# Routing searches with whole-array counts and broadcasts, 16-bit comparison tables with the token groups innermost, and high products first at the start of layer three

## The chip, the core and the metric

The kernel runs on one core of a Trainium2 chip. The metric is the device time of one execution in microseconds (us). TensorE (PE in the rows; PEld is its weight load) multiplies, VectorE is DVE, ScalarE is ACT, GpSimd is POOL, and SyncE (SP) issues most DMAs. The kernel before took 959.31 us, the median of three runs (948.09 to 986.38).

## What is computed

The reference runs three stages, cut here to what matters:

```python
# 1. attention, 4 x 8 heads, 576 positions, 64 wide -> x of 2304 tokens x 512 (pooled + local part)
# 2. expert routing and two layers (N, D, E, F = 2304, 512, 8, 1024; cap = 288)
logits = x @ w_gate
order = np.argsort(-logits.flatten())
for idx in order:                          # greedy: best score first
    tok, e = idx // E, idx % E
    if assigned[tok] >= 0 or counts[e] >= cap: continue
    assigned[tok] = e; counts[e] += 1
for e in range(E):
    h = np.maximum(x[assigned == e] @ w1[e], 0.0)
    out[assigned == e] = h @ w2[e]
# 3. two more layers (d_ff = 2048)
h = out @ w_in
g = np.maximum(h, 0.0) + alpha * np.minimum(h, 0.0)
return g @ w_out
```

## The kernel before

**Stages.** Attention fills the first 210 us. Then the router finds the expert that fills up first and the list of its 288 tokens, those rows of x are gathered, and a pass runs all four layers on them. There are eight passes, one for each expert in the order in which they fill. The routing for the first pass stands alone ahead of it; the routing for pass k + 1 is cut into pieces that stand between the matrix products of pass k (`pe_route` on TensorE, `dve_route` and `dve_prepare` on VectorE). The places are a fixed list of half steps (`PLACES`, `ROUTE`).

**Routing.** A token's best open score is a 32-bit key. The router searches for the score at which an expert fills in six levels of digits (5, 5, 5, 5, 6, 6 bits). At a level VectorE writes the table `at_least` (it lies in the buffer `onehot`): for each of 18 token groups and each of 32 or 64 candidate digits, is the token's digit at least this one (L1169). TensorE sums it over the 128 partitions, a **count** of 18 matmuls of bf16 with the weights `choice[:, t, :]`, 128 x 8 (L954), so the result has 8 rows, one per expert. VectorE compares the counts with the free places (`enough`, 8 rows, L1171), and a **broadcast**, one matmul with `ones[0:E, :]`, 8 x 128 (L957), tells all partitions how many experts have enough. VectorE adds this up (L1165) and forms the next place (L1166, L1167). After the levels come one count of everything (L959), two prefix sums (L962), and the **id list**: VectorE writes `onehot`, slot number against token, in two halves (L1234), and 18 matmuls with `onehot[:, t, :]`, 128 x 128, as weights give the token numbers (L965). In the routing that stands alone VectorE also makes the low halves of two resident weight units after each `at_least` (L1351).

**Passes.** Each float32 product is made from high and low halves: `three` issues high x high, low x high, high x low (L936 to L938); `two_by_high` issues the first two (L941, L942), `one_by_low` the third (L945). Layer one and two have 8 hidden blocks (288 columns), layer three and four 16 (256 columns, in passes 3 and 7 384 columns; passes are numbered from 0). Layer two's result y is copied by ScalarE (`y_hi`, L1442), and VectorE subtracts for the low half (`y_lo`, L1259), one chunk of four at a time. Block j of layer three (`pe_third`) goes into one of two PSUM banks. VectorE turns it into `act` in two operations (`dve_third`: `neg`, L1273, then `act`, L1275), ScalarE rounds it (L1446), VectorE makes the low half (`dve_third_low`, L1281), and `pe_fourth` adds the block into the outputs two steps later. Block j >= 2 of layer three waits for `act` of block j - 2. At the end of a pass blocks of 128 tokens are copied out of PSUM and scattered by GpSimd's indirect DMAs, one block after another (`dve_output`, `scatter`).

**Order around the change.** Engines work strictly in the order in which the functions issue. In step s of layers three and four TensorE's order is block s of layer three, a routing piece, block s - 2 of layer four, a routing piece. At s = 0 the piece is the count of the last level, at s = 1 its broadcast. VectorE's order at s = 0 is `neg`, `act` of block 0, then `enough`. Ahead of the four `y_lo` it has the last level's `at_least`.

## Time and profile before

| | before |
|---|---|
| median of three runs, us | 959.31 (948.09 to 986.38) |
| profiled execution, us | 948.44 |
| its span, us (first to last instruction) | 946.7 |
| mean granted TensorE clock, share of full | 0.941 |
| PE busy, us (share of the span) | 883.0 (93%) |
| PEld busy | 785.6 (83%) |
| DVE busy | 646.4 (68%) |
| ACT busy | 329.5 (35%) |
| POOL busy | 144.0 (15%) |
| PE in the chain of work that ended last | 86% |

In the page the span is cut into 40 slices of 23.7 us; a digit is the busy share of a slice in tenths, and PEclk is the clock that TensorE was granted, in tenths of full speed. A matmul's end in these profiles is modelled; what a stretch of matmuls costs is read from the starts of the ones around it.

### The profile page before, as it was taken

The page shows a single profiled execution, that of the slowest core. Times are in us where ns is not written, and L with a number is a line of the kernel's source. Part 1 is how long each engine was busy: PE and PEld are TensorE (multiplying, and loading weights), DVE is VectorE, ACT ScalarE, POOL GpSimd, SP SyncE. Part 2 cuts the span into 40 slices and gives each one's busy share as a digit, 9 for nine tenths or more (in the row PEclk, how much of TensorE's full clock was granted, in tenths as well). Part 3 has the DMA queues.
Part 4 walks back from the last instruction along what each step waited for, and adds up shares of the span by engine and source line. Part 5 has one row for each costly group of instructions (what it writes and reads, how often), then busy time and mean ns, then how long its engine had stood idle before and what let it go on. Part 6 is the DMA issues. An engine that isn't in the chain of part 4 may idle for free.

```text
span 946.7 us, 19340 instructions
## 1 busy us (share of the span) xinstructions
PE 883.0 (93%) x7228; PEld 785.6 (83%) x7228; DVE 646.4 (68%) x1818; ACT 329.5 (35%) x1041; POOL 144.0 (15%) x182
## 2 busy tenths in 40 slices
PE   7999999982299999999999999999999999999996
PEld 7688878771298889999899989898898998999995
DVE  4475858448778976877787766667777877775432
ACT  2666777733154143123214211331241142143111
POOL 4653736310100010010011001100100110020001
PEclk9589999775599999999999999999999999999998
DMA  7666471014453340212213020302122130231000
GB/s 161 150 145 173 103 173 49 19 52 134 136 166 114 100 141 2 89 55 90 90 35 113 1 90 26 111 13 90 52 90 85 37 112 1 90 109 37 1 1 34
DMA packets 122629, 77.29 MB, mean 82 GB/s; under 512 B 64232, under 2 KB 105192, under 8 KB 122536
## 3 DMA queue, kind: packets, MB, share of 16 engines
q1 hardware_dynamic: 119368, 65.83, 25.2%
q0 software_dynamic: 3168, 10.23, 3.4%
q8 instruction: 58, 0.95, 0.4%
q14 instruction: 35, 0.29, 0.1%
HBM read 66.59 MB, written 9.44 MB: 80 GB/s over the span
## 4 chain that ended last, share of the span: by engine, by line
PE 86%; DVE 7%; ACT 3%; issue 2%; DMA 1%; SPq 1%; POOL 0%; DVEq 0%; ACTq 0%; POOLq 0%
PE banks L936 22%; PE banks L937 20%; PE banks L938 20%; PE banks L954 3%; PE banks L258 3%; PE banks L307 2%; PE banks L359 2%; PE banks L270 2%; PE banks L330 2%; ACT prob L527 2%; PE banks L945 1%; PE banks L301 1%; PE banks L980 1%; PE banks L345 1%; PE banks L371 1%
## 5 line engine op out<-in xcount | busy, mean ns | idle before, releaser
L1446 ACT CAST hid<-act 128x256 fp32r<-128x256 f32 (+1 forms) x128 | 55.5, 434 | 326.5 <-DVE act L1275 326.5
L936 PE MATMUL banks<-xy,win 128*128 128x256 f32 (+1 forms) x480 | 143.9, 300 | 0.0
L938 PE MATMUL banks<-xy,win 128*128 128x256 f32 (+1 forms) x480 | 142.1, 296 | 0.0
L937 PE MATMUL banks<-xy,win 128*128 128x256 f32 (+1 forms) x480 | 142.0, 296 | 0.0
L1273 DVE TENSOR_SCALAR neg<-banks,alph 128x256 f32<-128x256 f32 (+1 forms) x128 | 66.1, 517 | 93.7 <-PE banks L938 81.5
L936 PE MATMUL banks<-wout,hid 128*128 128x512 f32 x288 | 116.2, 403 | 0.5 <-DVE hid L1281 0.5
L937 PE MATMUL banks<-wout,hid 128*128 128x512 f32 x288 | 113.4, 394 | 0.0
L938 PE MATMUL banks<-wout,hid 128*128 128x512 f32 x288 | 112.8, 392 | 0.0
L1481 POOL DMA_INDIRECT rows<-x_rows,id_new x24 | 23.2, 966 | 514.6 <-DVE id_new L1240 509.7
L936 PEld LDWEIGHTS banks<-xy,win 128*128 128x128 f32 x480 | 91.2, 190 | 4.9
L937 PEld LDWEIGHTS banks<-xy,win 128*128 128x128 f32 x480 | 91.2, 190 | 3.9
L527 ACT ACTIVATE prob<-banks,nbias 96x102 f32<-96x102 f32 (+1 forms) x256 | 85.9, 351 | 15.4 <-DVE nbias L444 8.1
L938 PEld LDWEIGHTS banks<-xy,win 128*128 128x128 f32 x480 | 91.1, 190 | 0.0
L936 PE MATMUL banks<-hid,w2s 128*128 128x288 f32 x256 | 79.8, 312 | 0.0
L937 PE MATMUL banks<-hid,w2s 128*128 128x288 f32 x256 | 75.3, 294 | 0.0
L938 PE MATMUL banks<-hid,w2s 128*128 128x288 f32 x256 | 75.2, 294 | 0.0
L588 POOL TENSOR_TENSOR prob<-prob,inverse 96x408 f32<-96x408 f32 (+1 forms) x80 | 61.2, 784 | 85.9 <-DVE inverse L461 85.9
L936 PE MATMUL banks<-xy,w1s 128*128 128x288 f32 x224 | 69.6, 311 | 0.1
L1351 DVE TENSOR_TENSOR w2s<-raw,w2s 128x512 fp32r<-128x512 f32 x64 | 44.0, 687 | 33.8 <-ACT w2s L1415 33.8
L937 PE MATMUL banks<-xy,w1s 128*128 128x288 f32 x224 | 66.6, 297 | 0.0
L938 PE MATMUL banks<-xy,w1s 128*128 128x288 f32 x224 | 66.5, 297 | 0.0
L938 PEld LDWEIGHTS banks<-wout,hid 128*128 128x128 f32 x288 | 54.1, 188 | 12.1
(202 smaller groups left out, 1892.9 us busy)
## 6 DMA issues: line engine op xcount, KB each, us to landing
raw<-in_moe_w SPq DMA_DIRECT2D x128, 256.0 KB, 3.3
qn<-in_q SPq DMA_DIRECT2D x48, 96.0 KB, 2.5
kn<-in_k SPq DMA_DIRECT2D x48, 96.0 KB, 2.5
vn<-in_v SPq DMA_DIRECT2D x4, 1152.0 KB
x_rows<-xs SPq DMA_DIRECT2D x24, 192.0 KB, 2.4
raw<-in_moe_w_in SPq DMA_DIRECT2D x16, 256.0 KB, 3.2
raw<-in_moe_w_out SPq DMA_DIRECT2D x16, 256.0 KB, 3.8
vw<-in_v SPq DMA_DIRECT2D x16, 204.0 KB
```

The lines of the kernel that those rows point to most:

```text
L258: nc.tensor.matmul(bank[:, 0:128], ident[:], ident[:], start=True, stop=True)
L270: last = nc.tensor.transpose(bank[:, x * T:(x + 1) * T], (qn, kn)[t][:, c * (R // 2) + x, 2 * hp:2 * hp + 2, :].rearrange("p h d -> p (h d)"),
L527: last = nc.scalar.activation(prob[0:rows, ring, at * width:(at + 1) * width], pS[u % 2][0:rows, g, n * width:(n + 1) * width], ACT.Exp, b ...
L588: nc.gpsimd.tensor_tensor(p, p, inv.unsqueeze(2).to_broadcast([rows, heads, width]), ALU.mult).then_inc(normed, 1)
L936: nc.tensor.matmul(out_ap, a_hi, b_hi, start=start, stop=False)
L937: nc.tensor.matmul(out_ap, a_lo, b_hi, start=False, stop=False)
L938: return nc.tensor.matmul(out_ap, a_hi, b_lo, start=False, stop=stop)
L954: last = nc.tensor.matmul(pR[0:E, 0:radix], choice[:, t, :], at_least[i // 2][:, t, :], start=(t == 0), stop=(t == NT - 1))
L1273: v.tensor_scalar(neg[:, 0:n], pH[j % 2][:, 0:n], 0.0, alph[:, j:j + 1], ALU.min, ALU.mult).then_inc(neg_made, 1)
L1351: v.tensor_tensor(unit_dst(n, resident, 1), raw[:, raw_slot(k, n)[0], :], unit_dst(n, resident, 0).bitcast(F32), ALU.subtract).then_inc(lo ...
L1446: nc.scalar.copy(hid[:, (FC + j) % 3, 0, 0:CHUNK[k]], act[:, j % 2, 0:CHUNK[k]]).then_inc(h_hi, 1)
L1481: nc.gpsimd.indirect_dma_start(out=rows[0:n, j, :], out_offset=None, in_=x_dram, in_offset=bass.IndirectOffsetOnAxis(ap=id_new[0:n, j:j + ...
```

## The change

- **Counts.** `choice` becomes the front of a wider, zero-filled buffer `choice_all`, and the weights of each count matmul are its 128 columns from t * E on: the first 8 are the group's, the other 120 give rows that nobody reads. The tile is 128 x 128 where it was 128 x 8.
- **Broadcasts.** `enough` has 128 rows, those behind the eighth zero, and the weights are all of `ones`: 128 x 128 where it was 8 x 128.
- **16-bit data, groups innermost.** `place`, the slot numbers (`slot16`), `any_v` and one table of numbers (`number`, 128 x 128 x 18) are bf16. `at_least` and `onehot` lie with the 18 groups innermost. So both inputs and the output of L1169 and L1234 are 16-bit with step 1, and TensorE reads `at_least[:, :, t]` (moving) and `onehot[:, :, t]` (weights) with a step of 18 elements, 36 bytes.
- **Layer three.** Blocks 0 and 1: the high products of both, then the low ones of block 0, the last count, the low ones of block 1.
- **`neg`** is written into `act` itself, so `dve_third` also waits for the low half of block j - 2.
- **Last pass.** The last two blocks of layer four are run together, token block by token block (`pe_fourth_last`).
- **Start.** The memsets of the routing's buffers move to the front of VectorE's program, with two new ones; VectorE waits for `logits` by semaphore. GpSimd fills `number` (2304 numbers a partition) where it filled 64 and 128.

```diff
-    f["digit_at"] = sb("digit_at", [T, J], F32)
-    f["slot_at"] = sb("slot_at", [T, SLOTS], F32)
+    f["number"] = sb("number", [T, SLOTS, NT], BF16)
...
-    choice = sb("choice", [T, NT, E], BF16)
+    choice_all = sb("choice", [T, NT * E + T - E], BF16)
...
-    place = sb("place", [T, 2, NT], F32)
-    enough = sb("enough", [E, J], BF16)
-    any_v = sb("any_v", [T, J], F32)
+    place = sb("place", [T, 2, NT], BF16)
+    slot16 = sb("slot16", [T, NT], BF16)
+    enough = sb("enough", [T, J], BF16)
+    any_v = sb("any_v", [T, J], BF16)
...
-    onehot = sb("onehot", [T, NT, SLOTS], BF16)
+    onehot = sb("onehot", [T, SLOTS, NT], BF16)
...
-                    last = nc.tensor.matmul(pR[0:E, 0:radix], choice[:, t, :], at_least[i // 2][:, t, :],
+                    last = nc.tensor.matmul(pR[:, 0:radix], choice_all[:, t * E:t * E + T], at_least[i // 2][:, :, t],
                                             start=(t == 0), stop=(t == NT - 1))
             else:
-                last = nc.tensor.matmul(pR[0:T, 0:radix], f["ones"][0:E, :], enough[:, 0:radix], start=True, stop=True)
+                last = nc.tensor.matmul(pR[0:T, 0:radix], f["ones"][:], enough[:, 0:radix], start=True, stop=True)
...
-                last = nc.tensor.matmul(pR[0:SLOTS, 0:2 * JT], onehot[:, t, :], ids[:, t].rearrange("p a b -> p (a b)"),
+                last = nc.tensor.matmul(pR[0:SLOTS, 0:2 * JT], onehot[:, :, t], ids[:, t].rearrange("p a b -> p (a b)"),
...
+    def pe_third_by_high(e, k, j):
+
+        e.wait_ge(h_lo, k * NC + FC + j + 1)
...
+            two_by_high(pH[j % 2][:, 0:CHUNK[k]], win[:, 0, j, c, :], win[:, 1, j, c, :], xy[:, 0, c, 0:CHUNK[k]], c == 0)
+
+    def pe_third_by_low(e, k, j):
...
+            last = one_by_low(pH[j % 2][:, 0:CHUNK[k]], win[:, 0, j, c, :], xy[:, 1, c, 0:CHUNK[k]], c == DC - 1)
+        last.then_inc(h_in_psum, 1)
...
+    def pe_fourth_last(e, k):
+
+        for i in range(BLOCKS[k]):
+            tokens = slice(i * SLOTS, (i + 1) * SLOTS)
+            for j in (FC2 - 2, FC2 - 1):
+                if i == 0:
+                    e.wait_ge(h_lo, k * NC + FC + j + 1 + 2)
+                r = (FC + j) % 3
+                last = three(pY[i], hid[:, r, 0, tokens], hid[:, r, 1, tokens], wout[:, 0, j, :], wout[:, 1, j, :],
+                             False, j == FC2 - 1)
+            last.then_inc(o_in_psum, 1)
...
-            if s < FC2:
+            if s == 0:
+                pe_third_by_high(e, k, 0)
+                pe_third_by_high(e, k, 1)
+                pe_third_by_low(e, k, 0)
+            elif s == 1:
+                pe_third_by_low(e, k, 1)
+            elif s < FC2:
                 pe_third(e, k, s)
...
-                each = [T, NT, radix]
-                ask(v.tensor_tensor(at_least[l], bc(here, 2, each), bc(f["digit_at"][:, 0:radix], 1, each), ALU.is_ge))
+                ask(v.tensor_tensor(at_least[l], bc(here, 1, [T, radix, NT]), f["number"][:, 0:radix, :], ALU.is_ge))
...
-            ins = v.tensor_tensor(onehot[:, h], bc(slot[:, h], 2, half), bc(f["slot_at"][:], 1, half), ALU.is_equal)
+            ins = v.tensor_tensor(onehot[:, h], bc(slot16[:], 1, [T, SLOTS // 2, NT]), f["number"][:, h], ALU.is_equal)
...
-        v.tensor_scalar(neg[:, 0:n], pH[j % 2][:, 0:n], 0.0, alph[:, j:j + 1], ALU.min, ALU.mult).then_inc(neg_made, 1)
+        e.wait_ge(h_lo, k * NC + FC + j + 1)
+        v.tensor_scalar(act[:, j % 2, 0:n], pH[j % 2][:, 0:n], 0.0, alph[:, j:j + 1], ALU.min, ALU.mult).then_inc(neg_made, 1)
```

TensorE's program at the start of layer three in pass 0, before: matmuls of layer three read `win`, the row with `choice` is the last count, the row with `enough` its broadcast; the high products of block 0 stand ahead of the first row.

```order
L942 MATMUL banks<-xy,win 128x256
L945 MATMUL banks<-xy,win 128x256 x4
L954 MATMUL banks<-onehot,choice 8x64 x18
L936 MATMUL banks<-xy,win 128x256
L937 MATMUL banks<-xy,win 128x256
L938 MATMUL banks<-xy,win 128x256
...
L957 MATMUL banks<-enough,ones 128x64
L936 MATMUL banks<-xy,win 128x256
```

The same place after the change, where the helper lines are one lower:

```order
L941 MATMUL banks<-xy,win 128x256
L944 MATMUL banks<-xy,win 128x256 x4
L953 MATMUL banks<-onehot,choice 128x64 x18
L944 MATMUL banks<-xy,win 128x256 x4
L956 MATMUL banks<-enough,ones 128x64
L935 MATMUL banks<-xy,win 128x256
```

Ahead of the count stand now 16 high products in place of 8, and between count and broadcast 4 matmuls in place of 12.

VectorE's program at a level of the routing that stands alone, a piece of before and the same piece of after; `win` and `wout` are the low halves of two resident weight units:

```order
L1169 TENSOR_TENSOR onehot<-place,digit_at 128x1152
L1351 TENSOR_TENSOR win<-raw,win 128x512
L1351 TENSOR_TENSOR wout<-raw,wout 128x512
L1171 TENSOR_SCALAR enough<-banks,cap 8x64
```

```order
L1195 TENSOR_TENSOR onehot<-place,number 128x1152
L1377 TENSOR_TENSOR win<-raw,win 128x512
L1377 TENSOR_TENSOR wout<-raw,wout 128x512
L1197 TENSOR_SCALAR enough<-banks,cap 8x64
```

Nothing has moved here: the two weight operations stand between the table and `enough` as before, and only the table's operands differ.

## Rows read from the trace of the kernel before

**Rows 1.** The page: the clock granted to TensorE in the 40 slices.

```profile
PEclk9589999775599999999999999999999999999998
```

**Rows 2.** Waits of TensorE, 205 to 262 us, then 262 to 946 us: total us, times, longest us.

```profile
PE banks L954 <- DVE onehot L1169: 14.9, 6, 5.8
...
PE banks L954 <- DVE onehot L1169: 0.6, 1, 0.6
```

**Rows 3.** Groups by line on VectorE: output<-inputs, shapes, count, busy us, mean ns.

```profile
L1169 DVE TENSOR_TENSOR onehot<-place,digit_at 128x576 bf16<-128x576 f32 x32 | 24.2, 756 | 0.9
L1169 DVE TENSOR_TENSOR onehot<-place,digit_at 128x1152 bf16<-128x1152 f32 x16 | 21.7, 1358 | 0.6
```

**Rows 4.** Timeline of the routing that stands alone, a 64-column count: start us, length us.

```profile
229.79 1.12 PE L954 MATMUL banks<-onehot,choice 128*8 128x64 bf16 x18 [2.17 <-DVE onehot L1169]
```

**Rows 5.** Timeline of TensorE in pass 1, around a 64-column count.

```profile
369.32 0.29 PE L938 MATMUL banks<-hid,w2s 128*128 128x288 f32 x1
369.60 0.69 PE L954 MATMUL banks<-onehot,choice 128*8 128x64 bf16 x18
...
370.45 0.29 PE L937 MATMUL banks<-hid,w2s 128*128 128x288 f32 x1
370.58 0.29 PE L938 MATMUL banks<-hid,w2s 128*128 128x288 f32 x1
```

**Rows 6.** Timeline of TensorE in pass 1, around a 32-column count.

```profile
357.70 0.29 PE L938 MATMUL banks<-hid,w2s 128*128 128x288 f32 x1
357.92 0.60 PE L954 MATMUL banks<-onehot,choice 128*8 128x32 bf16 x18
...
358.69 0.30 PE L937 MATMUL banks<-xy,w1s 128*128 128x288 f32 x1
```

**Rows 7.** Timeline of TensorE in pass 1, around bf16 pieces with 128 x 128 weights.

```profile
381.23 0.39 PE L938 MATMUL banks<-wout,hid 128*128 128x512 f32 x1
381.46 0.30 PE L959 MATMUL banks<-choice,ones 128*128 128x288 bf16 x1
...
381.71 0.28 PE L937 MATMUL banks<-xy,win 128*128 128x256 f32 x1
...
405.69 0.28 PE L938 MATMUL banks<-xy,win 128*128 128x256 f32 x1
405.81 0.61 PE L965 MATMUL banks<-ids,onehot 128*128 128x6 bf16 x18
...
406.59 0.39 PE L937 MATMUL banks<-wout,hid 128*128 128x512 f32 x1
```

**Rows 8.** Timeline of pass 1 where layer three begins, VectorE and TensorE.

```profile
372.98 1.36 DVE L1169 TENSOR_TENSOR onehot<-place,digit_at 128x1152 bf16<-128x1152 f32 x1
373.81 0.28 PE L941 MATMUL banks<-xy,win 128*128 128x256 f32 x1
374.26 1.54 DVE L1259 TENSOR_TENSOR xy<-banks,xy 128x288 fp32r<-128x288 f32 x4
374.80 1.44 PE L945 MATMUL banks<-xy,win 128*128 128x256 f32 x4
376.38 0.48 DVE L1273 TENSOR_SCALAR neg<-banks,alph 128x256 f32<-128x256 f32 x1 [0.32 <-PE banks L945]
377.24 0.26 DVE L1171 TENSOR_SCALAR enough<-banks,cap 8x64 bf16<-8x64 f32 x1
378.21 0.28 PE L938 MATMUL banks<-xy,win 128*128 128x256 f32 x1
378.42 0.20 PE L957 MATMUL banks<-enough,ones 8*128 8x64 bf16 x1
378.77 0.28 PE L937 MATMUL banks<-xy,win 128*128 128x256 f32 x1
```

**Rows 9.** Timeline of GpSimd at the end of the span: the first and the last scatter.

```profile
937.44 0.97 POOL L1491 DMA_INDIRECT out<-rows,id_now  x1 [89.87 <-DVE rows L1302]
...
940.00 0.97 POOL L1491 DMA_INDIRECT out<-rows,id_now  x1 [0.30 <-issue]
```

More of the change, by code:

```diff
@@ L727, in early_buffers, with experts @@
     alph = sb("alph", [128, FC2], F32)
-    return (open_l, best, pick, pick_n, choice, free, flip, key, digits_i, digits, place, enough, any_v, reach,
+    return (open_l, best, pick, pick_n, choice_all, free, flip, key, digits_i, digits, place, enough, any_v, reach,
             over_t, tie, choice2, taken, need, room, cap8, cap_d, penalty, full, fullest, sel, junk, expert_f,
-            expert_i, need1, mine, tied, upto, rowsum, rank, take, member, gone, mem, past, slot, in_tile, ids,
+            expert_i, need1, mine, tied, upto, rowsum, rank, take, member, gone, mem, past, slot, slot16, in_tile, ids,
             onehot, id_parts, id_f, id_new, id_now, id_left, raw, alph)
-def experts(nc, logits, w1, w2, w_in, w_out, alpha, x_dram, out, ident, f, early, consts_made, n_consts, TILE, SLOTS, psum, sem, sb, over):
+def experts(nc, logits, w1, w2, w_in, w_out, alpha, x_dram, out, ident, f, early, consts_made, n_consts, TILE, SLOTS, psum, sem, sb, over, logits_known):
     E, DM, F = w1.shape
@@ L750, in experts @@
     assert CAP * E == N and LEFT[E] == 0 and max(LEFT) + CAP <= WIDE <= 3 * SLOTS and min(BLOCKS) >= 2 and DM == 512 and FC % 2 == 0
-    J = f["digit_at"].shape[1]
+    J = 1 << max(DIGIT_BITS)
     LEVELS = len(DIGIT_BITS)
@@ L777, in experts @@
     hid = sb("hid", [128, 3, 2, WIDE], F32R)
-    neg = sb("neg", [128, WIDE], F32)
     act = sb("act", [128, 2, WIDE], F32)
     rows = sb("rows", [SLOTS, JT, DM], F32)
-    (open_l, best, pick, pick_n, choice, free, flip, key, digits_i, digits, place, enough, any_v, reach,
+    (open_l, best, pick, pick_n, choice_all, free, flip, key, digits_i, digits, place, enough, any_v, reach,
      over_t, tie, choice2, taken, need, room, cap8, cap_d, penalty, full, fullest, sel, junk, expert_f,
-     expert_i, need1, mine, tied, upto, rowsum, rank, take, member, gone, mem, past, slot, in_tile, ids,
+     expert_i, need1, mine, tied, upto, rowsum, rank, take, member, gone, mem, past, slot, slot16, in_tile, ids,
      onehot, id_parts, id_f, id_new, id_now, id_left, raw, alph) = early
     prod = pick
-    flat_onehot = onehot[:].rearrange("p t m -> p (t m)")
-    at_least = [flat_onehot[:, 0:NT * j].rearrange("p (t j) -> p t j", t=NT) for j in RADIX]
+    choice = choice_all[:, 0:NT * E].rearrange("p (t e) -> p t e", e=E)
+    flat_onehot = onehot[:].rearrange("p m t -> p (m t)")
+    at_least = [flat_onehot[:, 0:NT * j].rearrange("p (j t) -> p j t", t=NT) for j in RADIX]
     pH = [psum[0], psum[1]]
@@ L1016, in pe_second @@
             last.then_inc(h_used, 1)
[L1018 to L1024 removed]
+    def pe_third_by_high(e, k, j):
+        e.wait_ge(h_lo, k * NC + FC + j + 1)
+        if k == 0:
+            wait_low(e, None, 2 * j)
+        if j == 0 and LEFT[k] > 0:
+            e.wait_ge(left_hi, lefts_to(k))
+        for c in range(DC):
+            if j == 0:
+                e.wait_ge(y_hi, k * DC + c + 1)
+            two_by_high(pH[j % 2][:, 0:CHUNK[k]], win[:, 0, j, c, :], win[:, 1, j, c, :], xy[:, 0, c, 0:CHUNK[k]], c == 0)
+    def pe_third_by_low(e, k, j):
+        if j == 0 and LEFT[k] > 0:
+            e.wait_ge(left_lo, lefts_to(k))
+        for c in range(DC):
+            if j == 0:
+                e.wait_ge(y_lo, k * DC + c + 1)
+            last = one_by_low(pH[j % 2][:, 0:CHUNK[k]], win[:, 0, j, c, :], xy[:, 1, c, 0:CHUNK[k]], c == DC - 1)
+        last.then_inc(h_in_psum, 1)
+    def pe_third(e, k, j):
+        e.wait_ge(act_made, k * FC2 + j - 1)
+        if k == 0:
             wait_low(e, None, 2 * j)
         out_ap, y = pH[j % 2][:, 0:CHUNK[k]], xy[:, :, :, 0:CHUNK[k]]
[L1027 to L1039 removed]
+        for c in range(DC):
+            last = three(out_ap, win[:, 0, j, c, :], win[:, 1, j, c, :], y[:, 0, c, :], y[:, 1, c, :], c == 0, c == DC - 1)
         last.then_inc(h_in_psum, 1)
@@ L1076, in pe_pass @@
                 pe_turn(e, k + 1, 1)
-            if s >= DELAY:
+            if s >= DELAY and (more or s < SECOND - 2):
                 pe_fourth(e, k, s - DELAY)
+            if not more and s == SECOND - 2:
+                pe_fourth_last(e, k)
             if more and at + 1 in pe_piece:
@@ L1352, in dve_weights, with vector_begin @@
                         ALU.subtract).then_inc(lo_by_dve, 1)
-    def vector(e):
-        e.sem_inc(h_lo, 2)
+    def vector_begin(e):
+        v.memset(enough[:], 0.0).then_inc(begun, 1)
+        v.memset(choice_all[:], 0.0).then_inc(begun, 1)
         v.memset(free[:], 1.0).then_inc(begun, 1)
```

56 lines of the change are left out of this document (21 added, 35 removed).

## The prediction

> **What bounds the kernel now.** I read the slices of the page first, then TensorE's waits, then the timeline of one pass. The page gives TensorE 93% of the span and 86% of the chain that ended last. Its clock stands at half (1.2 of 2.4 GHz) in the two slices of the routing that stands alone, and at full from there on [rows 1]. In that stretch TensorE waits for VectorE: six waits of 14.9 us in all for the tables of the six levels. From 262 us to the end the same wait occurs once, with 0.6 us [rows 2]. So there are two regimes. In the routing that stands alone, some 48 us, VectorE's chain of operations sets the time. In the eight passes, 676 us, TensorE has no gap, and every piece that stands between the products costs what it takes on TensorE. What it takes is read from the starts of the products around it, since a matmul's modelled length overlaps with the next.
>
> **The counts and broadcasts in the passes.** Products of 288 columns start 0.13 us apart, those of 256 columns 0.12 and those of 512 columns 0.23 [rows 5, 7, 8]. Around a 64-column count the product before starts at 369.32 and the second one behind it at 370.45: 1.13 us, less two steps of 0.13, leaves 0.87 us for the piece [rows 5]. A 32-column count costs 358.69 - 357.70 - 0.26 = 0.73 us [rows 6]. A broadcast, one matmul of 64 columns, costs 378.77 - 378.21 - 0.24 = 0.32 us [rows 8]. The pieces whose tile is already 128 x 128 are much cheaper: one bf16 matmul of 288 columns costs 381.71 - 381.23 - 0.23 - 0.12 = 0.13 us, and the 18 of the id list 406.59 - 405.69 - 0.12 - 0.23 = 0.55 us [rows 7]. Both are bf16 between float32 products and start without a gap, so the extra is not due to the type; the broadcast has the same 128 columns of weights and only 8 rows, so what it has in common with the counts is a tile smaller than the array. I take the price after from these pieces. Broadcast: 0.13, a gain of 0.19. 32-column count: 18 matmuls as in the id list, 0.56, a gain of 0.17. 64-column count: 0.09 more, the difference of the two counts' lengths of 0.69 and 0.60 [rows 5, 6], so 0.64, a gain of 0.23. Routing is mixed into seven passes, with four small counts, two large ones and six broadcasts each: 28 x 0.17 + 14 x 0.23 + 42 x 0.19 = 4.8 + 3.2 + 8.0 = 16.0 us. The bound on the good side is a count with nothing but its columns. The one on the bad side is the new step of 36 bytes, which no row shows. The nearest row is the same count at half the clock, 1.12 us for 18 [rows 4], against 0.69 [rows 5]: if the strided read ran at half rate, a large count would cost 0.43 more, and a small one, whose 32 columns then take no longer than 64 do now, 0.09 at most. I take no penalty, since the rows nearest in form (18 matmuls, 128 x 128) are of the packed kind and nothing in them is bound by reading.
>
> The Trainium skill speaks against this (Advanced Engine Details and Errata, section SBUF Cachelines): at least two accesses must hit a line of 16 bytes for full rate, and a step of 36 bytes gives one. By that rule the large counts would keep little of their gain; no row here has such a step on TensorE.
>
> **The tables on VectorE.** `at_least` takes 0.756 us for 576 elements and 1.358 for 1152 [rows 3]. The difference is 0.602 for 576, so the fixed part is 0.154. With 16-bit data throughout it lies between the fixed part and today's price; no row of `tensor_tensor` has only 16-bit operands. I take the middle, half the price per element: 0.455 and 0.756, a gain of 0.30 and 0.60. In the routing that stands alone these are on the path. At level 0 the gain is lost, and with it that of the memsets that move to the front: `enough` stands there behind weight units that wait for their DMA. Levels 1 to 3 give 3 x 0.30, since the small count is shorter than the two weight operations behind the table. Levels 4 and 5 give 2 x 0.60 if the large count stays at its 1.12 us [rows 4]: it starts earlier with the table and ends about when the two weight operations do, as now. The two halves of `onehot`, of the larger shape, give 1.2. Sum 3.3 us. If the clock rises at the same instant as now although the first pass starts 3.3 us sooner, half of it goes again: bounds 1.7 and 3.3, none at all if 16-bit data are no faster. In pass 0 the one wait for a table [rows 2] goes: 0.6 us. In the other passes a faster table is worth nothing by itself, since TensorE does not wait for it.
>
> The Trainium skill (VectorE: DVE Perf Modes, section The perf-mode tier table) has `tensor_tensor` on bf16 in SBUF at two elements a cycle. By that page the two tables would take about 0.46 and 0.76 us, an estimate, and the gain would be the same.
>
> **Layer three.** Before, TensorE starts the high products of block 0 at 373.81, its low ones at 374.80, and they last 1.44 us to 376.24 in place of four steps, because `y_lo` runs only from 374.26 to 375.80, behind the last table of 1.36 us. `neg` starts 0.14 us behind the last low product, `enough` 0.86 us behind `neg`, takes 0.26, and the broadcast starts at 378.42 [rows 8]. After: high products of both blocks to 374.80 + 0.96 = 375.76, the last of four low ones starts at 376.12 and ends at 376.40, 0.16 later than now; `neg` 376.54, `enough` 377.40 to 377.66, the broadcast about 377.72. TensorE itself would be ready at 375.76 + 0.48 + 0.64 + 0.48 = 377.36. So the wait on `y_lo` goes and a new wait of 0.4 us for `enough` comes. The broadcast is 0.70 earlier, of which the count's 0.23 is booked already: 0.45 us in each of six passes, 2.7 us. In pass 3, with 384 columns, the chain behind block 0 is longer by two operations of 128 more columns, 0.27 us, and little was waited for: I take -0.2. Pass 7 has no routing: block 2 waits for `act` of block 0. That is ready 1.0 us behind the end of block 0's last product, as `enough` is ready to start [rows 8], 0.1 more until `act` has ended, 0.27 for the columns and 0.16 for the product's own end; four products of 0.17 cover 0.7 of the 1.5 us: -0.8 us. Sum 1.7 us; bounds -1 and 4. What a faster table does here is hidden: with `y_lo` 0.6 us sooner the old order would have lost its stall too, so the new order by itself is then worth less than nothing, some 0.3 us a pass.
>
> **The rest.** In the last pass the first token block is complete after 6 of the last 18 products where it was after 12: 6 x 0.23 = 1.4 us earlier. The three scatters are issued one after another, 1.28 us apart, from 937.44 to 940.00 [rows 9], so the last issue moves as far as the first, unless its own copy, which does not move, holds it: I take 1.2 us, an estimate (bounds 0 and 1.4). `neg` in place and its wait cost nothing: the operation it waits for stands just ahead of it on VectorE, which mostly waits for TensorE there. The memsets and the longer fill of `number`, some 2 us of GpSimd, lie in the first microseconds, where VectorE and GpSimd wait for inputs.
>
> **Sum.** 16.0 + 3.3 + 0.6 + 1.7 + 1.2 = 22.8 us, against the profiled execution's 948.44: 925.6, I say 926 us. The median of the runs shown lies 1.1% above that execution and its lowest run at 948.09; the sum is for an execution like the profiled one, and the range's upper part has to hold a median that lies higher.
>
> **The rivals.**
> - *The strided reads run at half rate.* For it: the step lets each element be read alone, where two stand together now. Against it: pieces of 18 matmuls take 0.55 us for 6 columns and 0.73 for 32, so columns are hardly what bounds them [rows 6, 7]. It costs 14 x 0.43 = 6.0 us in the large counts, and if the weights of the id list load at half rate too, about 0.45 us in each of eight, 3.6 us: 935 us. Chance 0.28.
> - *16-bit data are no faster on VectorE*, because of the repeated row of `place`: 3.3 and 0.6 us are lost, 929.5 us. Chance 0.10.
> - *The new wait in layer three is longer than 0.4 us*, because `act` and `enough` come later than worked out. At 1 us more in each pass: 934 us. Chance 0.07.
> - *Slower than before.* The place is TensorE's read with the 36-byte step, in all 42 counts and 7 id lists of the passes. The gain is gone when each costs 22.8 / 49 = 0.47 us more, that is 26 ns a matmul, twice the present step; slower by 2% needs 0.85 us each. A half rate does not do this to the small counts. Chance 0.05.
>
> **How the numbers follow.** My forecast has 0.50. Its own range is 920 to 931, by the bounds of the terms. Half rate ends at 935 and the longer wait at 934, and a median above an undisturbed execution adds up to 1%, so the range is 918 to 940. A measurement of this kernel can tell about 2% from no change. Faster by over 2% means below 929.5: most of the forecast (0.42) and a part of the VectorE and half-rate cases (0.08), 0.50. Slower by over 2%: 0.04. Within: 0.46.
>
> **What would show it.** A broadcast piece should cost 0.13 us between the starts around it, a small count 0.56, a large one 0.64, and a pass of 256 columns should be 2.7 us shorter. The tables should take 0.46 and 0.76 us. TensorE should wait 0.4 us for `enough` ahead of the last broadcast, and 0.8 us in the last pass ahead of block 2. I am wrong if the count pieces are as dear as now (the step), if the tables keep 0.76 and 1.36 us, or if the pieces with a full tile owe their low price to something else.

## The result

The changed kernel takes 980.44 us (median of 4 runs, 975.75 to 983.91); the kernel before, on the same chip, 960.55 (4 runs, 948.09 to 986.38). The ratio is 1.025 with a 95% interval of 1.014 to 1.036: slower, though not surely by over 2%, where 926 us and a gain had been forecast. Ratios and intervals here leave out executions over 1.5% above the fastest of their kernel; medians leave out none. The profiled execution took 983.91 us, the longest of the four, with a span of 982.2 us, 35.5 us more than the span before.

The page of the changed kernel: engines, and the granted clock in 40 slices.

```profile
span 982.2 us, 19390 instructions
PE 921.4 (94%) x7228; PEld 835.7 (85%) x7228; DVE 621.7 (63%) x1820; ACT 331.2 (34%) x1041; POOL 146.7 (15%) x181
PEclk9595988975589999999999999999999999999999
```

Groups of the changed kernel by line, engine and shape (count, then busy us, mean ns of one, idle ahead): the count, its weights, the id list, its weights; and the tables on VectorE.

```profile
L953 PE MATMUL banks<-onehot,choice 128*128 128x32 bf16 x576 | 39.9, 239 | 9.0 <-DVE onehot L1195 9.0
L953 PE MATMUL banks<-onehot,choice 128*128 128x64 bf16 x288 | 36.2, 295 | 3.4 <-DVE onehot L1195 3.4
L964 PE MATMUL banks<-ids,onehot 128*128 128x6 bf16 x144 | 10.2, 204 | 3.7 <-DVE onehot L1259 3.7
...
L964 PEld LDWEIGHTS banks<-ids,onehot 128*128 128x128 bf16 x144 | 9.6, 160 | 4.2 <-DVE onehot L1259 3.8 <-issue 0.2
...
L1195 DVE TENSOR_TENSOR onehot<-place,number 128x576 bf16<-128x576 bf16 x32 | 14.6, 456 | 0.9
L1195 DVE TENSOR_TENSOR onehot<-place,number 128x1152 bf16<-128x1152 bf16 x16 | 12.1, 758 | 0.5
```

The tables came out as forecast, 456 and 758 ns where [rows 3] has 756 and 1358. The counts did not, as TensorE's timeline of pass 1 shows: a small count, a large count, an id list (start us, length us). They answer to [rows 5] to [rows 8].

```profile
381.36 0.29 PE L937 MATMUL banks<-xy,w1s 128*128 128x288 f32 x1
381.49 1.25 PE L953 MATMUL banks<-onehot,choice 128*128 128x32 bf16 x18
...
382.76 0.29 PE L936 MATMUL banks<-hid,w2s 128*128 128x288 f32 x1
...
387.39 0.29 PE L937 MATMUL banks<-hid,w2s 128*128 128x288 f32 x1
387.52 2.26 PE L953 MATMUL banks<-onehot,choice 128*128 128x64 bf16 x18
...
389.76 0.29 PE L936 MATMUL banks<-hid,w2s 128*128 128x288 f32 x1
...
425.19 0.28 PE L937 MATMUL banks<-xy,win 128*128 128x256 f32 x1
425.31 1.28 PE L964 MATMUL banks<-ids,onehot 128*128 128x6 bf16 x18
...
426.78 0.39 PE L936 MATMUL banks<-wout,hid 128*128 128x512 f32 x1
```

By starts, as before: the large count costs 389.76 - 387.39 - 0.26 = 2.11 us (0.87 before, 0.64 forecast), the small one 382.76 - 381.36 - 0.26 = 1.14 (0.73, 0.56), the id list 426.78 - 425.19 - 0.12 - 0.23 = 1.24 (0.55, unchanged by the forecast). The broadcasts cost 0.12 to 0.13 on average, as forecast. Against a packed full tile, a pass then pays 4 x 0.59 + 2 x 1.47 + 0.69 = 6.0 us more.

**Where the time lies.** The routing that stands alone begins with `open_l` at 210.93 us before and at 224.74 after, although nothing ahead of it was changed but memsets, the fill of `number` and one wait. VectorE's timeline, before, then after:

```profile
210.93 0.31 DVE L1122 TENSOR_TENSOR open_l<-logits,penalty 128x144 f32<-128x144 f32 x1
```

```profile
224.74 0.31 DVE L1149 TENSOR_TENSOR open_l<-logits,penalty 128x144 f32<-128x144 f32 x1
```

So 13.8 of the 35.5 us lie ahead of all that the change is about, and from this start to the end of the span it is 735.8 us before and 757.5 after, 21.7 more. I use this "rest" for all kernels below; it repeats within 0.4 us in the three kernels that were profiled twice. Between kernels it is less sharp: e6's pieces cost what the changed kernel's do, and its passes 1 to 6 agree to 0.05 us, yet its routing and pass 0 together take 2.9 us more (138.3 against 135.4), for which no cause was found. A price is therefore read from passes 1 to 6. Stages, us:

| kernel | routing begins | first product behind it | pass 1 | pass 3 | last pass, to its last matmul | rest |
|---|---|---|---|---|---|---|
| before | 210.9 | +47.0 | 79.99 | 101.44 | 92.64 | 735.8 |
| e4 (before again) | 210.4 | +47.8 | 79.99 | 101.44 | 92.67 | 735.8 |
| changed | 224.7 | +48.8 | 83.02 | 104.88 | 93.56 | 757.5 |
| e10 (changed again) | 216.3 | +48.2 | 83.01 | 104.88 | 93.62 | 757.1 |
| e1, packed (2 bytes) | 212.5 | +48.7 | 77.68 | 99.72 | 93.58 | 722.3 |
| e2, pairs (4 bytes) | 213.7 | +44.6 | 77.34 | 99.38 | 93.58 | 714.1 |
| e9 (6 bytes) | 238.1 | +46.3 | 77.67 | 99.70 | 93.58 | 719.0 |
| e5 (12 bytes) | 230.4 | +46.5 | 80.69 | 102.58 | 93.62 | 738.6 |
| e6 (18 bytes) | 218.7 | +49.3 | 83.01 | 104.89 | 93.60 | 760.5 |
| e7, 36 bytes, narrow tile | 221.9 | +48.6 | 84.40 | 106.35 | 93.61 | 767.6 |
| e3, broadcasts alone | 225.9 | +47.9 | 79.19 | 100.60 | 92.65 | 731.3 |
| e8, pairs, old layer three | 226.3 | +45.2 | 77.28 | 98.93 | 92.67 | 713.6 |
| e12 (e8 again) | 230.9 | +45.5 | 77.26 | 98.93 | 92.67 | 713.4 |
| e11, e8 and old last groups | 205.6 | +45.7 | 77.29 | 98.93 | 92.66 | 714.8 |

### The profile page after: what moved, and what is told of

It is laid out like the page before. It is cut to its first block, busy times and chain, and to the rows that moved or that the text cites. A ratio compares the mean times of both kernels' runs of the same rounds, so it can differ in the third digit from the quotient of the medians.

```text
span 982.2 us, 19390 instructions
## 1 busy us (share of the span) xinstructions
PE 921.4 (94%) x7228; PEld 835.7 (85%) x7228; DVE 621.7 (63%) x1820; ACT 331.2 (34%) x1041; POOL 146.7 (15%) x181
## 4 chain that ended last, share of the span: by engine, by line
PE 84%; SPq 6%; DVE 3%; DMA 2%; ACT 2%; issue 1%; POOL 0%; ACTq 0%; POOLq 0%; DVEq 0%
PE banks L935 20%; PE banks L936 19%; PE banks L937 19%; PE banks L953 7%; SPq L201 4%; PE banks L359 2%; PE banks L307 2%; SPq L211 2%; PE banks L330 2%; PE banks L940 1%; PE banks L270 1%; PE banks L258 1%; PE banks L941 1%; PE banks L944 1%; ACT prob L527 1%
## 5 line engine op out<-in xcount | busy, mean ns | idle before, releaser
L935 PE MATMUL banks<-xy,win 128*128 128x256 f32 (+1 forms) x448 | 133.7, 299 | 0.6 <-DVE act L1301 0.6
L1299 DVE TENSOR_SCALAR act<-banks,alph 128x256 f32<-128x256 f32 (+1 forms) x128 | 66.2, 517 | 107.2 <-PE banks L937 85.3
L937 PE MATMUL banks<-xy,win 128*128 128x256 f32 (+1 forms) x448 | 132.8, 296 | 0.0
L936 PE MATMUL banks<-xy,win 128*128 128x256 f32 (+1 forms) x448 | 132.6, 296 | 0.0
L935 PEld LDWEIGHTS banks<-xy,win 128*128 128x128 f32 x448 | 85.2, 190 | 5.1 <-DVE act L1301 0.9
L936 PEld LDWEIGHTS banks<-xy,win 128*128 128x128 f32 x448 | 85.1, 190 | 3.9
L953 PE MATMUL banks<-onehot,choice 128*128 128x32 bf16 (+1 forms) x864 | 76.1, 257 | 12.4 <-DVE onehot L1195 12.4
L937 PEld LDWEIGHTS banks<-xy,win 128*128 128x128 f32 x448 | 85.1, 190 | 0.0
L953 PEld LDWEIGHTS banks<-onehot,choice 128*128 128x128 bf16 x864 | 65.9, 116 | 16.1 <-DVE onehot L1195 8.0
L935 PE MATMUL banks<-xy,w1s 128*128 128x288 f32 x224 | 68.7, 307 | 0.1
L936 PE MATMUL banks<-xy,w1s 128*128 128x288 f32 x224 | 66.2, 296 | 0.0
```

Source lines behind the costliest of these rows:

```text
L935: nc.tensor.matmul(out_ap, a_hi, b_hi, start=start, stop=False)
L936: nc.tensor.matmul(out_ap, a_lo, b_hi, start=False, stop=False)
L937: return nc.tensor.matmul(out_ap, a_hi, b_lo, start=False, stop=stop)
L953: last = nc.tensor.matmul(pR[:, 0:radix], choice_all[:, t * E:t * E + T], at_least[i // 2][:, :, t], start=(t == 0), stop=(t == NT - 1))
L1299: v.tensor_scalar(act[:, j % 2, 0:n], pH[j % 2][:, 0:n], 0.0, alph[:, j:j + 1], ALU.min, ALU.mult).then_inc(neg_made, 1)
```

## Experiments: the step of the reads

Theory: the 36-byte step makes TensorE's reads dear, moving data and weights. Rival: the whole-array tile itself costs it.

**e1_packed**: the changed kernel with the groups outermost again, so that reads are packed; the tables then have a repeated input.

```diff
-    onehot = sb("onehot", [T, SLOTS, NT], BF16)
+    onehot = sb("onehot", [T, NT, SLOTS], BF16)
...
-                    last = nc.tensor.matmul(pR[:, 0:radix], choice_all[:, t * E:t * E + T], at_least[i // 2][:, :, t],
+                    last = nc.tensor.matmul(pR[:, 0:radix], choice_all[:, t * E:t * E + T], at_least[i // 2][:, t, :],
...
-                last = nc.tensor.matmul(pR[0:SLOTS, 0:2 * JT], onehot[:, :, t], ids[:, t].rearrange("p a b -> p (a b)"),
+                last = nc.tensor.matmul(pR[0:SLOTS, 0:2 * JT], onehot[:, t, :], ids[:, t].rearrange("p a b -> p (a b)"),
```

> The changed kernel with one part undone: the tables lie as before, the candidates of a group side by side, so TensorE reads them packed; 16-bit data, whole-array counts and broadcasts and all else stay. Theory S (the step of 36 bytes costs, 1.75 ns a column): a small count falls from 1.15 to about 0.56 us, a large one from 2.11 to about 0.64, the id list from 1.24 to 0.55; a pass of 256 columns takes 77.3 us (83.0 in the changed kernel, 80.0 before), and the kernel is about 19 us faster than before. Theory W (the wide tile itself costs, by its 128 weight columns or 128 result rows): counts stay at 1.15 and 2.11 us and passes near 82.5. The tables on VectorE go back to 0.76 and 1.36 us under both, since one input then repeats one element.

**e2_groups_of_two**: the table in pairs of groups. The reads have a step of 2 elements, 4 bytes, and VectorE has runs of two equal neighbours in all its operands. e9_step6, e5_step12 and e6_step18 are the same with 3, 6 and 9 in place of 2.

```diff
+    onehot = sb("onehot", [T, NT // 2, SLOTS, 2], BF16)
...
+                    last = nc.tensor.matmul(pR[:, 0:radix], choice_all[:, t * E:t * E + T], at_least[i // 2][:, t // 2, :, t % 2],
...
+                last = nc.tensor.matmul(pR[0:SLOTS, 0:2 * JT], onehot[:, t // 2, :, t % 2], ids[:, t].rearrange("p a b -> p (a b)"),
...
+                each = [T, NT // 2, radix, 2]
+                ask(v.tensor_tensor(at_least[l], bc(here.rearrange("p (a g) -> p a g", g=2), 2, each), bc(f["number"][:, 0:radix, :], 1, each), ALU.is_ge))
```

> The changed kernel with another table layout: groups in pairs, [9 pairs][candidates][2], so TensorE reads with a step of 4 bytes where it was 36, and VectorE still has two elements side by side everywhere. If what costs is the distance (a new piece of memory for each column), counts cost 0.56 and 0.64 us, the id list 0.55, tables still 0.46 and 0.76 us, and the kernel is some 22 us faster than before. If every step but one element costs alike, counts stay at 1.15 and 2.11 us and the time at that of the changed kernel. Anything between says how the price grows with the step.

Measured: e1 943.74 us, ratio 0.986 (0.979 to 0.991); e2 928.64, ratio 0.979 (0.965 to 0.993). TensorE's timeline of e2 in pass 1, the small count, the large one and the id list:

```profile
342.21 0.29 PE L937 MATMUL banks<-xy,w1s 128*128 128x288 f32 x1
342.35 0.61 PE L953 MATMUL banks<-onehot,choice 128*128 128x32 bf16 x18
...
343.02 0.29 PE L936 MATMUL banks<-xy,w1s 128*128 128x288 f32 x1
...
363.98 0.29 PE L937 MATMUL banks<-hid,w2s 128*128 128x288 f32 x1
364.11 0.71 PE L953 MATMUL banks<-onehot,choice 128*128 128x64 bf16 x18
...
364.88 0.29 PE L936 MATMUL banks<-hid,w2s 128*128 128x288 f32 x1
...
399.20 0.28 PE L937 MATMUL banks<-xy,win 128*128 128x256 f32 x1
399.32 0.61 PE L964 MATMUL banks<-ids,onehot 128*128 128x6 bf16 x18
...
400.10 0.39 PE L936 MATMUL banks<-wout,hid 128*128 128x512 f32 x1
```

That is 0.55, 0.64 and 0.55 us, the forecast's 0.56, 0.64 and 0.55. With the same full tile as in the changed kernel the counts are cheap again, and by the whole of what was lost: 83.02 - 77.34 = 5.68 us a pass, where the pieces make 6.0 and a wait for `enough`, which e2 has and the changed kernel hardly, takes the 0.3 between them (below). In e1 the tables take 757 and 1358 ns again, as dear as in [rows 3], so both things are shown: on 16-bit data a repeated input keeps VectorE at the old price, and pairs are enough for the new one. Its large count waits 0.34 us for its table. Its passes of 77.68 us came near the 77.3 expected, but its rest is 13.5 us shorter than before and not 19: the old tables cost in the routing too.

One group of e1, the 64-column table on VectorE:

```profile
L1195 DVE TENSOR_TENSOR onehot<-place,number 128x1152 bf16<-128x1152 bf16 x16 | 21.7, 1358 | 0.6
```

VectorE's groups of e2, the tables and the two parts of the slot table:

```profile
L1196 DVE TENSOR_TENSOR onehot<-place,number 128x576 bf16<-128x576 bf16 x32 | 14.6, 456 | 0.9
L1196 DVE TENSOR_TENSOR onehot<-place,number 128x1152 bf16<-128x1152 bf16 x16 | 12.1, 758 | 0.6
L1262 DVE TENSOR_TENSOR onehot<-slot,number 128x1280 bf16<-128x1280 bf16 x8 | 6.6, 819 | 0.0
L1262 DVE TENSOR_TENSOR onehot<-slot,number 128x1024 bf16<-128x1024 bf16 x8 | 5.5, 685 | 0.0
```

**e7_narrow_tile**: the changed kernel with the 36-byte step, but the old count tile of 128 x 8.

```diff
-                    last = nc.tensor.matmul(pR[:, 0:radix], choice_all[:, t * E:t * E + T], at_least[i // 2][:, :, t],
+                    last = nc.tensor.matmul(pR[0:E, 0:radix], choice_all[:, t * E:t * E + E], at_least[i // 2][:, :, t],
```

> The changed kernel with the counts' tile back to 128 x 8 and the step of 36 bytes kept. If the moving read alone costs (1.75 ns a column), a large count stays at 18 x 0.117 = 2.1 us and gets the 0.25 us of the switch of tiles on top, some 2.35 us, a small one 1.4. If the 128 columns of weights take part in the price, the counts get cheaper than 2.11 and 1.15 us.

TensorE's timeline of e7, pass 1, the large count:

```profile
387.10 0.29 PE L937 MATMUL banks<-hid,w2s 128*128 128x288 f32 x1
387.33 2.26 PE L953 MATMUL banks<-onehot,choice 128*8 128x64 bf16 x18
...
389.75 0.30 PE L936 MATMUL banks<-hid,w2s 128*128 128x288 f32 x1
```

Measured: 991.26 us in one execution; the large count costs 2.39 us and the small one 1.36. The narrow tile is dearer by 0.28 and 0.22 us at the 36-byte step too, a little over the 0.23 and 0.17 that the forecast gave the full tile. The rival falls: the tile brought its gain, and the step took it and more.

**How the price goes with the step.**

> The changed kernel with groups in sixes, [3][candidates][6]: TensorE reads with a step of 12 bytes. At 4 bytes a large count costs 0.63 us, at 36 bytes 2.11. Theory L (the price comes from how many columns lie in one stretch of 16 bytes: four at a step of 4, one and a third at 12, one at 36): a large count near the dear end, 1.5 to 2.1 us. Theory D (the price grows evenly with the distance): 0.63 + 8/32 of 1.48 = 1.0 us, a small count 0.70.

> The changed kernel with groups in nines, [2][candidates][9]: a step of 18 bytes. Theory L: every column lies in a stretch of its own, so the price is that of 36 bytes: 2.1 us for a large count, 1.15 for a small one, 1.24 for the id list. Theory D: 0.63 + 14/32 of 1.48 = 1.28 us for a large count. The tables have rows of nine, an odd number; if VectorE still takes two at a time they stay at 0.46 and 0.76 us.

> The changed kernel with its tables in groups of three of the 18: the values that one count matmul reads stand 6 bytes apart (2 bytes in e1_packed, 4 in e2_groups_of_two, 12 in e5_step12, 18 in e6_step18, 36 in the changed kernel). Prices so far at 4, 12 and 18 bytes, from starts around the piece: small count 0.55, 0.90, 1.15 us; large count 0.63, 1.60, 2.13 us; id list 0.55, 0.95, 1.18 us. By the stretch theory (what costs is the number of 16-byte stretches that a row of the read touches, 1.85 ns each, 2.13 us over 18 x 64, and nothing beyond the floor of the packed piece): 3 of 8 values open a new stretch, so the large count takes 18 x 64 x 3/8 x 1.85 ns = 0.80 us, the small one 0.40 us by stretches and so its floor of 0.55 us, the id list its floor of 0.55 us. By the distance theory (an even rise from 4 to 18 bytes): large 0.84, small 0.64, id list 0.64 us. The small count and the id list tell them apart.

Measured: 970.74, 980.88 and 958.81 us for 12, 18 and 6 bytes, one execution each, so with all the chance of the attention stage. By the starts around the pieces, in us (middle of the pieces that started without a wait):

| step, bytes | small count, 576 values | large count, 1152 | id list, 2304 weights | rest |
|---|---|---|---|---|
| 2 | 0.55 | 0.62 | 0.55 | 722.3 |
| 4 | 0.55 | 0.63 | 0.55 | 714.1 |
| 6 | 0.55 | 0.88 | 0.58 | 719.0 |
| 12 | 0.90 | 1.60 | 0.95 | 738.6 |
| 18 | 1.15 | 2.13 | 1.18 | 760.5 |
| 36 | 1.14 | 2.11 | 1.24 | 757.5 |

The rest is not the step's alone: at 2 bytes the tables are slow (e1), and at 6 and 18 bytes their rows of 3 and 9 are odd. VectorE's tables of e9, then of e6:

```profile
L1196 DVE TENSOR_TENSOR onehot<-place,number 128x1152 bf16<-128x1152 bf16 x16 | 15.3, 958 | 0.6
```

```profile
L1196 DVE TENSOR_TENSOR onehot<-place,number 128x1152 bf16<-128x1152 bf16 x16 | 13.2, 825 | 0.6
```

With rows of 2, 6 and 18 they take 758 ns. Less the forecast's fixed 154 ns, 958 is 4/3 and 825 is 10/9 of that: an odd row costs what the next even one does, so e6's tables did not stay at 0.76 us.

The large count at 12 and at 6 bytes, in TensorE's timelines of e5, then of e9:

```profile
386.85 0.29 PE L937 MATMUL banks<-hid,w2s 128*128 128x288 f32 x1
386.98 1.74 PE L953 MATMUL banks<-onehot,choice 128*128 128x64 bf16 x18
...
388.72 0.29 PE L936 MATMUL banks<-hid,w2s 128*128 128x288 f32 x1
```

```profile
391.49 0.29 PE L937 MATMUL banks<-hid,w2s 128*128 128x288 f32 x1
391.63 0.97 PE L953 MATMUL banks<-onehot,choice 128*128 128x64 bf16 x18
...
392.63 0.29 PE L936 MATMUL banks<-hid,w2s 128*128 128x288 f32 x1
```

The price rises from 12 to 18 bytes and no further to 36, so it is not the distance. It goes with the number of 16-byte stretches that a row of the read touches: one for each value at 18 and 36 bytes, 3/4 at 12, 3/8 at 6. With stretches of 8 bytes the price at 12 would be that at 36, with 32 bytes that at 18 would lie below it; neither is so. Between the small and the large count at 18 bytes lie (2.13 - 1.15) / 576 = 1.7 ns for each value, which leaves 0.17 us for the piece. Then 12 bytes give 0.17 + 0.75 x 1.96 = 1.64 (measured 1.60) and 0.91 (0.90), and 6 bytes 0.91 (0.88), while at 4 bytes the stretches come to 0.66, about what a packed piece costs anyhow (0.62). The count's price at 12 and 18 bytes fits the stretches and not an even rise; at 6 bytes e9's expectation of 0.80 for the large count was 0.08 too low since it left the fixed part out, but the small count stayed at 0.55, where an even rise would have given 0.64. The id list, whose strided operand is the weights, behaves alike at a lower price, with the same 0.17 us taken off (1.24 - 0.17) / 2304 = 0.46 ns a stretch. The Trainium skill (Advanced Engine Details and Errata, section SBUF Cachelines) has SBUF in lines of 16 bytes that need at least two hits each; the trace agrees with the line's size. By the two-hit rule a 6-byte step, with two or three hits a line, would be free; the large count at 0.88 against 0.63 is not.

At half the clock it is, as the large counts of e9 and e2 in the routing show (granted clock 0.50 in both):

```profile
257.04 1.14 PE L953 MATMUL banks<-onehot,choice 128*128 128x64 bf16 x18 [1.77 <-DVE onehot L1196]
```

```profile
231.55 1.14 PE L953 MATMUL banks<-onehot,choice 128*128 128x64 bf16 x18 [1.57 <-DVE onehot L1196]
```

Both last 1.14 us there, 0.97 and 0.71 in the passes, while e5's lasts 1.74 in both places. So what a count costs here is the longer of two things: its columns, which go with the clock, and its stretches, which do not.

## Experiments: what else the change did

**e3_broadcast_only**: the kernel before, with nothing but the whole-array broadcasts.

```diff
-    enough = sb("enough", [E, J], BF16)
+    enough = sb("enough", [T, J], BF16)
...
-                last = nc.tensor.matmul(pR[0:T, 0:radix], f["ones"][0:E, :], enough[:, 0:radix], start=True, stop=True)
+                last = nc.tensor.matmul(pR[0:T, 0:radix], f["ones"][:], enough[:, 0:radix], start=True, stop=True)
```

> The kernel before with the broadcasts alone made 128 x 128. If a tile smaller than the array costs the switch, the piece falls from 0.32 to 0.13 us, passes of 256 columns from 80.0 to 78.9 us, and the span's part behind the first product by about 8 us. If the low price of the full pieces came from something else, it stays at 0.32 us and 80.0 us.

**e4_before_again**: the kernel before, unaltered, beside it.

> The kernel before once more, for its attention stage. In the changed kernel's profile the routing began at 224.7 us, in that of before at 210.9. If this is chance (where the clock of TensorE falls to half in attention), this run's start of the routing may lie anywhere from 210 to 225 us, and kernels with the new start of the program may lie anywhere there too. If it is the changed start (memsets and the longer table fill ahead of attention), it stays at about 211 here and at about 224 in the two kernels that keep the new start.

Measured: 958.95 and 947.97 us, one execution each. The broadcast costs 0.13, and pass 1 is 0.80 us shorter, not 6 x 0.19 = 1.1: the large count in it, at 1.05 us by its starts, now waits 0.33 us for its table, as in e1. So the rest is 4.5 us shorter and not 8, and e3 still took longer than e4, since its routing began at 225.9 and not 210.4.

**e10_after_again**: the changed kernel once more, for that start.

> The changed kernel once more, unaltered. The stand-alone routing began at 210.9 us in the profile of the kernel before and at 224.7 us in that of the changed one, with the same attention code ahead of it. If the 13.8 us are chance of the execution (which stretches of attention run at the half clock), the routing begins anywhere between 210 and 231 us here, as it did over the runs so far, while the seven passes and the last one repeat theirs to 0.2 us each but pass 0 (83.0 a pass, 104.9 for pass 3, 93.6 the last). If they belong to the changed program, it begins at 224 to 225 us again.

Measured: 975.16 us. The routing began at 216.27, passes 1 to 6 repeated to 0.03 us and the last one to 0.06. Over all the profiles it began anywhere between 205.6 and 238.1, for one kernel (e8, e12) at 226.3 and 230.9. The granted clock of e11 and of e9, the two ends:

```profile
PEclk9589999995599999999999999999999999999998
```

```profile
PEclk9569556999559999999999999999999999999998
```

Ahead of the routing's own two slices at half clock (5), e11 has one and e9 three, with two more partly so (6). A slice is 23 to 24 us. Kernels with the old start of the program lie as far apart (210.4 and 225.9 for e4 and e3) as those with the new one. So the 13.8 us are chance of the execution, and what decides how much of attention runs at half clock was not settled. That this is also most of the spread of the executions without a trace is likely, not shown.

**e8_pairs_old_third**: e2 with layer three in its old order.

```diff
-            if s == 0:
-                pe_third_by_high(e, k, 0)
-                pe_third_by_high(e, k, 1)
-                pe_third_by_low(e, k, 0)
-            elif s == 1:
-                pe_third_by_low(e, k, 1)
+            if s in (0, 1):
+                pe_third_by_high(e, k, s)
+                pe_third_by_low(e, k, s)
```

> Groups in pairs, and the start of layer three as before: block 0 whole, count, block 1 whole. The prediction said that with a faster table the new order is worth less than nothing, 0.3 us a pass and 0.8 us in the last pass. By that the passes of 256 columns take 77.0 us (77.3 with the new order), the stretch from the last pass's first product to its last matmul 92.7 (93.6), and the whole is 2.5 to 3 us faster than the kernel with pairs and the new order. If the new order does what it is for, this run is slower, by up to 0.45 us a pass. Either way it is the candidate for the fastest: 925 us where an undisturbed run of before takes 948, ratio 0.976.

**e11_old_third_old_last** takes the old last groups as well (`pe_fourth_last` gone), and **e12_best_again** is e8 once more.

> e8_pairs_old_third with the last layer-four groups back in their old place too, so that of the change only the whole-array counts and broadcasts and the 16-bit tables (in pairs, 4 bytes apart) are left. My theory of the end: with the old order the last matmul starts 9.7 us ahead of the span's end as in the kernel before, and with the new one 8.5, the gain of 1.2 us that the prediction gave it; passes unchanged at 77.2 to 77.3 us and the last pass at 92.7. By the rival (the end is given by the last scatter whatever the order) the two kernels have the same distance from last matmul to end. In the whole time the two differ by 1.2 us of 930, which the timed rounds cannot tell.

> e8_pairs_old_third once more, beside e11: passes 77.2 to 77.3 us, last pass 92.7 us, last matmul 8.5 us ahead of the end, whatever the attention stage takes this time. The time against the kernel before: a ratio of 0.97 again, from 20 us less in the passes.

Measured: e8 930.44 us (6 runs), ratio 0.971 (0.966 to 0.977); e12 940.32 (4 runs), ratio 0.981 (0.968 to 0.995); e11 941.65 (4 runs, 922.15 to 966.01). TensorE's waits in e2's passes (266 to 920 us), then in the last pass alone:

```profile
PE banks L956 <- DVE enough L1198: 2.6, 7, 0.7
PE banks L935 <- DVE act L1304: 0.6, 1, 0.6
```

The new order has its wait for `enough`, 0.37 us on average (0.4 forecast), and in the last pass 0.6 us for `act` ahead of block 2; the same view of the kernel before has no wait for `act` from 262 us on. Against the old order of e8, passes 1, 2, 4 and 5 are 0.05 to 0.19 us longer, pass 6 is 0.46 longer, pass 3 0.45 and the last pass 0.91, 2.2 us in all. e8 had been expected 2.5 to 3 us ahead of e2; its rest is only 0.5 us shorter, since its routing and pass 0 take 1.6 us more (127.1 against 125.5). Of these, 0.65 lie in the routing that stands alone, which is the same in both, so at least in part they are chance. The old order no longer stalls with the faster table: in e11's timeline `y_lo` starts at 361.62, as the first high product does (at 361.66), where in [rows 8] it starts 0.45 us behind it, and the low products go with 0.18 us of wait.

```profile
361.62 1.55 DVE L1282 TENSOR_TENSOR xy<-banks,xy 128x288 fp32r<-128x288 f32 x4
...
362.64 0.96 PE L944 MATMUL banks<-xy,win 128*128 128x256 f32 x4
363.22 0.19 PEld L944 LDWEIGHTS banks<-xy,win 128*128 128x128 f32 x1 [0.18 <-DVE xy L1282]
363.45 0.71 PE L953 MATMUL banks<-onehot,choice 128*128 128x64 bf16 x18
```

At the end, GpSimd's last scatter in e11, then in e2:

```profile
913.69 0.97 POOL L1521 DMA_INDIRECT out<-rows,id_now  x1 [0.30 <-issue]
```

```profile
921.11 0.97 POOL L1526 DMA_INDIRECT out<-rows,id_now  x1 [0.30 <-issue]
```

The last matmul starts at 910.68 in e11 and 919.28 in e2, so the scatter stands 3.01 us behind it in the old order, as before, and 1.83 in the new: 1.18 us, the forecast's 1.2.

## Why the prediction was wrong

The sum had five terms; e2 differs from the changed kernel only in how the tables lie, so it measures them one by one. `neg` in place and the new start of the program were booked at nothing; they stand in all variants of the changed kernel and were not tested by themselves.

- **Broadcasts and full tiles, 16.0 us: the price of the tile was right, that of the step was the failed step.** With a 4-byte step each piece costs what the forecast took. The sentence that failed is "I take no penalty, since the rows nearest in form (18 matmuls, 128 x 128) are of the packed kind and nothing in them is bound by reading". Those rows have no strided read in them, so they could not speak for it. The penalty is 0.59 us a small count, 1.47 a large one and 0.69 an id list: 28 x 0.59 + 14 x 1.47 + 7 x 0.69 = 41.9 us in the passes, of which 39.1 show (first product to last matmul 700.1 us against 661.0 in e2), 0.4 a pass being hidden, since the dear last count leaves hardly any wait for `enough` (its broadcast costs 0.17 there against 0.60 in e2).
- **The rivals had the cause and not its size.** Half rate was priced at 0.43 us on a large count, from a count at half the clock. But that row says what a column costs at half the clock, not what a slow read costs. (For its 0.45 us on an id list it names no row; measured are 0.69.) The changed kernel's large count lasts 2.27 us in the routing, at half the clock, and 2.26 in pass 1, at full: these reads do not go with TensorE's clock. At 1.7 ns a value, against 0.46 ns for a column of the products (0.13 us for 288), they run at about a quarter of the rate. The rival "slower than before" had the right place and asked for 0.47 us in each of 49 pieces; the mean was 0.86, past even the 0.85 that it named for slower by 2%. It was put aside by "a half rate does not do this to the small counts" at 0.05. With a small count at 18 x 32 values and no row with such a step, a multiple of the column's time should have been carried as an open bound, and with the rule that spoke against the change this chance should have been several times larger.

The large count in the routing, changed kernel:

```profile
243.86 2.27 PE L953 MATMUL banks<-onehot,choice 128*128 128x64 bf16 x18 [1.57 <-DVE onehot L1195]
```

- **Tables, 3.3 us.** 456 and 758 ns are the forecast's 0.455 and 0.756. From the start of the routing to the first product, the four profiles with pairs (e2, e8, e12, e11) have 44.6, 45.2, 45.5 and 45.7 us against 47.0 and 47.8: 1.3 to 3.2 us, mostly inside the bounds of 1.7 to 3.3 and under the 3.3 taken. In the changed kernel the counts took it back (48.8). That TensorE does not wait for the tables in the other passes held for the old pieces alone: once the broadcasts are cheap, the old table costs 0.34 us a pass (e1, e3). So 7 x 0.34 = 2.4 of the 16.0 us need the faster tables, which the sum did not say. Of the 0.6 us booked for pass 0's wait for a table, e2 still waits 0.2.
- **Layer three, 1.7 us.** Its balance came out in e2: passes 0 to 6 and the last pass are 18.1 us shorter than before (17.4 against e4), where 16.0 + 0.6 + 1.7 = 18.3 had been forecast, with both new waits near their sizes. But the gain isn't the order's. As the forecast said in its last sentence there, the faster table removes the old stall by itself; then the new order is worth -0.17 us in the mean of passes 1, 2, 4, 5 and 6 (-0.3 had been guessed), -0.45 in pass 3 and -0.91 in the last.
- **End, 1.2 us**: 1.18.
- **Sum.** 22.8 us had been forecast. e2's rest is 21.7 us shorter, e8's and e12's 22.2 and 22.4. The changed kernel's is 21.7 us longer. Part of this agreement is luck, since the routing and pass 0 of e2 and e8 differ by 1.6 us. The step alone, and not one of the other terms, turned the sign. (The eight passes before last 679.1 us and not the prediction's 676, and TensorE does wait 1.5 us in all behind 262 us; neither changes the sum.)

e8 beats both kernels: 2.9% under the one before by its own executions, 1.9% by those of its repeat e12, and 2.4% by the rest (22.2 and 22.4 of 946.7 us). Only its own interval, which ends at 0.977, lies wholly beyond 2%. It has whole-array tiles and 16-bit tables with the groups in pairs, and layer three as it was.

## What to carry to other kernels

Choose a table's layout for the engine that reads it on the path, and look for one that both can have: pairs of 16-bit values gave VectorE its full gain and left TensorE's reads at the price of packed ones. When the trace has no row with the access pattern that a change brings in, the missing price is an open bound and not zero; a small kernel that measures it alone is worth more than the rest of the sum. And undo parts one by one even where the sum fits: a reordering got credit here for a stall that a faster operation had removed.

## What the hardware showed that I had not expected

- A bf16 read of TensorE whose values stand 18 or 36 bytes apart takes about 1.7 ns a value as moving data and 0.46 ns as weights, at 12 bytes 3/4 of it, at 4 bytes nothing over packed; the length is the same at either clock (2.27 and 2.26 us). At 6 bytes a count of 18 x 64 values costs 0.25 us more at full clock and nothing more at half.
- A matmul with a tile of 128 x 8 or 8 x 128 between full ones costs 0.18 to 0.28 us once for the piece, whatever the number of matmuls in it: 0.19 for a single broadcast, 0.18 to 0.28 for the 18 of a count.
- On VectorE a bf16 `tensor_tensor` whose rows are odd takes each row as if it had one element more: 758 ns for 1152 elements in rows of 2, 6 or 18, 825 in rows of 9, 958 in rows of 3; with an input repeated inside the row it takes 1358.
- The same attention code, ahead of the routing, took from 205.6 to 238.1 us, with one to three of its slices at half clock and up to two partly. These 32.5 us are more than the whole effect of the change (21.7); the rest, measured from the start of a stage behind it, repeated to 0.4 us where a kernel was profiled twice.
